# The last tile's output product with tokens on the partitions, in four banks, stored as rows of 1 KB

## What is computed

```python
X = np.fft.rfft(x, axis=1)
Yr = Xr @ w_r - Xi @ w_i + b_r
Yi = Xr @ w_i + Xi @ w_r + b_i
# each of both: sign(Y) * max(|Y| - 0.01, 0)
y = np.fft.irfft(Yr + 1j * Yi, n=3008, axis=1).reshape(12032, 256)
h = y @ w_in                                # 256 -> 2048
g = np.maximum(h, 0) + alpha * np.minimum(h, 0)
out = g @ w_out                             # 2048 -> 256
```

## Time and profile before

| | |
|---|---|
| median of 3 runs | 1376.64 us (1376.47 to 1377.29) |
| profiled execution, its own time | 1377.65 us |
| its span | 1375.8 us |
| TensorE busy | 1358.3 us, 99% of the span |
| VectorE, ScalarE, POOL busy | 1028.1, 765.3, 327.2 us |
| mean granted TensorE clock | 0.998 of full speed |

### The profile page before, as it was taken

How to read it: one execution, slowest core, us unless ns; L and a number is a source line. 1 busy time by engine, 2 the same in 40 slices (tenths; PEclk the granted TensorE clock), 3 DMA queues, 4 the chain that set the end, 5 groups by cost and what they waited for, 6 DMA issues and landing times.

```text
span 1375.8 us, 21743 instructions
## 1 busy us (share of the span) xinstructions
PE 1358.3 (99%) x6933; PEld 1157.8 (84%) x6933; DVE 1028.1 (75%) x1891; ACT 765.3 (56%) x1711; POOL 327.2 (24%) x370
## 2 busy tenths in 40 slices
PE   7999999999999999999999999999999999999997
PEld 5998888888888888888888888888888888888886
DVE  7877788898866768989866668888886666566654
ACT  4875566666544555655644546666564444444443
POOL 4534442232201422323300332233220000000000
PEclk9999999999999999999999999999999999999999
DMA  8754523231221541323302333223211021102101
GB/s 263 186 169 131 176 61 93 68 96 50 52 51 41 148 114 56 87 69 82 80 29 50 89 110 80 81 66 83 83 43 44 26 50 39 25 26 50 27 15 16
DMA packets 174892, 106.82 MB, mean 78 GB/s; under 512 B 112438, under 2 KB 150582, under 8 KB 174779
## 3 DMA queue, kind: packets, MB, share of 16 engines
q1 hardware_dynamic: 170340, 101.58, 27.6%
q10 hardware_dynamic: 3959, 3.70, 0.8%
q0 software_dynamic: 480, 0.16, 0.1%
HBM read 67.89 MB, written 37.49 MB: 77 GB/s over the span
## 4 chain that ended last, share of the span: by engine, by line
PE 96%; DVE 2%; DMA 1%; ACT 1%; issue 0%; POOL 0%; POOLq 0%; SPq 0%; DVEq 0%; ACTq 0%
PE out_ps L546 40%; PE h_ps L546 39%; PE work_ps L546 11%; PE work_ps L648 2%; PE work_ps L580 2%; PE work_ps L650 1%; PE work_ps L581 1%; DVE x_lo L1050 1%; DMA pair_raw<-fwd_scratch 1%; DVE x_hi L1058 0%; ACT above L881 0%; DMA x_raw<-in_x_dram 0%; DMA fwd_scratch<-g_raw 0%; DVE shrunk L1120 0%; ACT shr_hi L887 0%
## 5 line engine op out<-in xcount | busy, mean ns | idle before, releaser
L920 ACT ACTIVATE rows<-h_ps 128x502 f32<-128x502 f32 (+1 forms) x384 | 225.7, 588 | 509.8 <-PE h_ps L546 509.8
L1151 DVE SCALAR_TENSOR_TENSOR g_raw<-rows,keep,h_ps 128x502 f32<-128x502 f32 (+1 forms) x384 | 280.2, 732 | 264.3 <-ACT rows L920 260.4
L546 PE MATMUL out_ps<-g_hi,wout_hi 128*128 128x502 f32 (+1 forms) x768 | 305.0, 397 | 0.1
L546 PE MATMUL h_ps<-y_hi,win_hi 128*128 128x502 f32 (+1 forms) x768 | 300.4, 391 | 0.9 <-DVE y_lo L1050 0.9
L546 PE MATMUL h_ps<-y_lo,win_hi 128*128 128x502 f32 (+1 forms) x768 | 300.4, 391 | 0.0
L546 PE MATMUL out_ps<-g_hi,wout_lo 128*128 128x502 f32 (+1 forms) x768 | 299.8, 390 | 0.0
L546 PE MATMUL h_ps<-y_hi,win_lo 128*128 128x502 f32 (+1 forms) x768 | 299.5, 390 | 0.0
L546 PE MATMUL out_ps<-g_lo,wout_hi 128*128 128x502 f32 (+1 forms) x768 | 299.0, 389 | 0.0
L1050 DVE TENSOR_TENSOR g_lo<-g_raw,g_hi 128x502 fp32r<-128x502 f32 (+1 forms) x384 | 268.9, 700 | 1.8 <-ACT g_hi L929 1.4
L929 ACT ACTIVATE g_hi<-g_raw 128x502 fp32r<-128x502 f32 (+1 forms) x384 | 237.1, 617 | 6.6 <-DVE g_raw L1151 6.2
L546 PEld LDWEIGHTS h_ps<-y_hi,win_hi 128*128 128x128 f32 x768 | 145.4, 189 | 31.4 <-issue 1.0
(11 more groups left out here) (174 smaller groups left out, 2024.9 us busy)
## 6 DMA issues: line engine op xcount, KB each, us to landing
pair_raw<-fwd_scratch SPq DMA_DIRECT2D x96, 128.0 KB, 2.2
rows<-inv_scratch SPq DMA_DIRECT2D x61, 192.0 KB, 2.5
table<-in_twiddles_dram SPq DMA_DIRECT2D x28, 384.0 KB, 3.5
inv_scratch<-inv_sb SPq DMA_DIRECT2D x36, 256.0 KB, 2.2
x_raw<-in_x_dram SPq DMA_DIRECT2D x56, 160.0 KB
fwd_scratch<-staging SPq DMA_DIRECT2D x46, 192.0 KB, 2.1
inv_sb<-inv_scratch SPq DMA_DIRECT2D x122, 64.0 KB, 2.3
out_dram<-turned SPq DMA_DIRECT2D x124, 40.0 KB, 1.8
```

Source lines behind the costliest of these rows:

```text
L546: mm = pe.matmul(ps, lhs, rhs, start=(first and n == 0), stop=(last and n == len(terms) - 1), **kw)
L920: act.activation(negpart[:, q % 2, 0:size], h_ps[:, q % 2, 0:size], ACT.Relu, scale=-1.0).then_inc(negpart_done, 1)
L1151: dve.scalar_tensor_tensor(g_raw[:, q % 2, 0:size], negpart[:, q % 2, 0:size], keep[:, m:m + 1], h_ps[:, q % 2, 0:size], ALU.mult, ALU.add ...
```

## The change

Only the last tile's output product, its way out of the banks and its stores are changed. In `output_last` the weights of the array are blocks of g (124, 128, 128 and 120 tokens, by LAST_AT) and the moving operand is w_out, 256 features wide. So the tokens lie on the partitions and a token's 256 features in a row. Four banks collect the four blocks: the two of `out_ps` and the first two of `work_ps`. A step has twelve matmuls of 256 columns instead of six of 500. The wait for `g_lo` stands inside the first block, before its third matmul; the first two need `g_hi` alone. The waits for tile 22's transposes are at block 0 and block 1, and block 2 waits for the last reading of `work_ps` by the first layer.

Each block has its own signal in the last step. VectorE copies blocks 0 and 2, ScalarE blocks 1 and 3, into the place that `turned` has for this tile; there are no transposes for it. Eight transfers store whole rows of 1 KB, one transfer for each stretch of a block with one value of b: 30 and 94 rows (block 0, SP), 94 and 34 (block 1, POOL), 60 and 68 (block 2, SP), 26 and 94 (block 3, ScalarE).

```diff
+LAST_AT = (0, 124, 252, 380, 500)
+LAST_BLOCKS = len(LAST_AT) - 1
...
+def last_runs():
+    runs = []
+    for j in range(LAST_BLOCKS):
+        at = LAST_AT[j]
+        while at < LAST_AT[j + 1]:
+            b, a = divmod(TILE_AT[2][0] + at, NA)
+            count = min(NA - a, LAST_AT[j + 1] - at)
+            runs.append((j, at - LAST_AT[j], count, b, a))
+            at += count
+    return runs
...
+        out_rows_v = out.rearrange("(g a b) d -> g a b d", a=NA, b=NB)
...
+        def last_bank(j):
+            return out_ps[:, j, 0:DIM] if j < 2 else work_ps[:, j - 2, 0:DIM]
...
+        def store_last(eng, n, landed):
+            j, at, count, b, a = last_runs()[n]
+            eng.wait_ge((last_even, last_odd)[j % 2], j // 2 + 1)
+            eng.dma_start(out_rows_v[BATCH - 1, a:a + count, NB // 2 + b, :],
+                          last_place(j)[at:at + count, :]).then_inc(landed, 16)
...
-            for n in (0, 2, 4, 6):
-                store_out(sp, TILES - 1, n)
+            for n in (0, 1, 4, 5):
+                store_last(sp, n, last_stored)
...
-                sp.wait_ge(out_stored[k], 16 * (12 * TILES // 2 - 3 * k))
-            sp.wait_ge(out_handed, 16 * 3)
+                sp.wait_ge(out_stored[k], 16 * 12 * (TILES // 2 - k))
+            sp.wait_ge(last_stored, 16 * 6)
+            sp.wait_ge(out_handed, 16 * 2)
...
+            def output_last(m):
+                q = (TILES - 1) * STEPS + m
+                pe.wait_ge(g_hi_done, q + 1)
+                for j in range(LAST_BLOCKS):
+                    at = slice(LAST_AT[j], LAST_AT[j + 1])
+                    ps = last_bank(j)[0:LAST_AT[j + 1] - LAST_AT[j], :]
+                    gh, gl = g_hi[:, q % 3, at], g_lo[:, q % 3, at]
+                    hi, lo = wout_hi[:, m // 2, m % 2, :], wout_lo[:, m // 2, m % 2, :]
+                    if m == 0 and j < 2:
+                        pe.wait_ge(turned_done, 2 * (TILES - 1) - 1 + j)
+                    if m == 0 and j == 2:
+                        pe.wait_ge(biased_done, PAIRS * BATCH)
+                    product(ps, [(gh, hi), (gh, lo)], first=m == 0, last=False)
+                    if j == 0:
+                        pe.wait_ge(g_lo_done, q + 1)
+                    mm = product(ps, [(gl, hi)], first=False, last=m == STEPS - 1)
+                    if m == STEPS - 1:
+                        mm.then_inc(last_mm, 1)
+                if m < STEPS - 1:
+                    mm.then_inc(out_mm, 1)
...
-            for n in (1, 3, 5, 7, 8):
-                store_out(act, TILES - 1, n)
+            for j in range(1, LAST_BLOCKS, 2):
+                act.wait_ge(last_mm, j + 1)
+                act.wait_ge(out_stored[(TILES - 1) % 2], 16 * 12 * ((TILES - 1) // 2))
+                rows_of = slice(0, LAST_AT[j + 1] - LAST_AT[j])
+                act.activation(last_place(j)[rows_of, :], last_bank(j)[rows_of, :], ACT.Copy).then_inc(last_odd, 1)
+            for n in (6, 7):
+                store_last(act, n, last_stored)
...
-            turn(TILES - 1, 0)
-            turn(TILES - 1, 1)
+            for j in range(0, LAST_BLOCKS, 2):
+                dve.wait_ge(last_mm, j + 1)
+                dve.wait_ge(out_stored[(TILES - 1) % 2], 16 * 12 * ((TILES - 1) // 2))
+                rows_of = slice(0, LAST_AT[j + 1] - LAST_AT[j])
+                dve.tensor_copy(last_place(j)[rows_of, :], last_bank(j)[rows_of, :]).then_inc(last_even, 1)
...
-            for n in (9, 10, 11):
-                store_out(pool, TILES - 1, n, out_handed)
+            for n in (2, 3):
+                store_last(pool, n, out_handed)
```

More of the change, by code:

```diff
@@ L250, in mixer_kernel @@
         head_loaded, out_handed = sem("head_loaded"), sem("out_handed")
+        last_mm, last_even, last_odd, last_stored = (sem(n) for n in ("last_mm", "last_even", "last_odd", "last_stored"))
         ffw_loaded = [sem(f"ffw_loaded_{k}") for k in range(2)]
@@ L348, in mixer_kernel, with store_out @@
         wout_v = w_out.rearrange("(m p) e -> p m e", p=P)
+        out_rows_v = out.rearrange("(g a b) d -> g a b d", a=NA, b=NB)
         out_v = out.rearrange("(g a b) (h q e) -> g q a b h e", a=NA, b=NB, h=DH, q=4)
-        def store_out(eng, f, n, landed=None):
+        def store_out(eng, f, n):
             g, q, (k, b, count) = f // 6, n % 4, TILE_STORES[f % 3][n // 4]
@@ L357, in store_out, with last_place @@
                          turned[32 * q:32 * q + rows, f % 2, k, at:at + count, :, :].rearrange("p b h e -> p (b h) e")
-                         ).then_inc(landed or out_stored[f % 2], 16)
+                         ).then_inc(out_stored[f % 2], 16)
+        def last_bank(j):
+            return out_ps[:, j, 0:DIM] if j < 2 else work_ps[:, j - 2, 0:DIM]
+        def last_place(j):
+            return turned[:, (TILES - 1) % 2, :, :, :, :].rearrange("p k b h e -> p (k b h e)")[:, j * DIM:(j + 1) * DIM]
+        def store_last(eng, n, landed):
[3 more added lines that the diff above has]
+                          last_place(j)[at:at + count, :]).then_inc(landed, 16)
         def store_fwd(eng, s):
@@ L789, in _ @@
                     q = f * STEPS + m - LAG
-                    if q >= 0:
+                    if q >= (TILES - 1) * STEPS:
+                        output_last(q % STEPS)
+                    elif q >= 0:
                         output(*divmod(q, STEPS))
             for m in range(STEPS - LAG, STEPS):
-                output(TILES - 1, m)
+                output_last(m)
         @block.scalar
```

## The result

The changed kernel takes 1379.73 us (1378.97 to 1381.22, 14 runs), the kernel before 1377.47 us in the same jobs (1376.37 to 1378.41, 14 runs). The ratio is 1.0018, 95% interval 1.0011 to 1.0025: slower by 2.5 us (1.5 to 3.4). The forecast was +0.65 us, "no difference", and a time of 1377.3 in a range up to 1379.6.

A forecast was written before the change was run, and what follows sets the result against it. TensorE, busy 99%, bounds the kernel until the tail. The last data run starts 0.1 us sooner (+1.05 of longer steps paid back) and lasts +0.8: +0.65 after rounding on 1376.64 gives 1377.3 us, range 1374.3 to 1379.6.

The forecast's parts named there:

- The product: Last tile's output product: twelve 256-column matmuls take 1.43 us against 1.357, +0.075 a step, 13 steps +1.0 us, +0.05 at tile start.
- The handover to step 15: Before the last output product: the present 0.25 us wait for g_lo goes and nothing takes its place.
- Copies: Out of the banks: ScalarE 0.37 us and VectorE 0.42 us a copy; last block out 0.47 later, block 0 0.55 earlier.
- issues: Tail stores: an issue takes about 0.45 us on SP and ScalarE and 0.7 on POOL.
- The deal of the rows: Tail stores on SP and ScalarE: rows go to engines in equal shares, so 94 rows mean two engines with 47 each.
- the rival without it (1374.5): Tail stores: the 94-row stores are dealt over all 16 engines, 2.1 us sooner, 1374.5 us; chance 0.14.
- The price of a row: Tail data: 0.045 us a row, upper bound 0.055; 117 rows keep the first two engines busy 5.3 us, to 1375.2.
- POOL's rows: Tail stores: the main case (chance 0.58) counts only SP's and ScalarE's 119 rows on the first two engines, none of POOL's.
- the rival (+2.1): POOL's 94 rows fall on the same two engines, 47 more rows: +2.1 us, 1379.4, up to 1380.5; chance 0.22.
- The end: After the last data: landing comes 0.5 us behind and the span's end 0.75 later, as in the kernel before.
- the stretch at a low share: Sign in the tail: data moving at an eighth of 16 engines for some 4 us after 1371, where it was near nine.
- SP's last wait: Sign at the end: SP's wait for the last landing is around 5 us, against 4.0 in the kernel before.

The follow-up runs named there:

- The split version: The changed kernel with every 94-row store issued as 80 + 14 rows, eleven stores in place of eight: 1375.99 us, ratio to the kernel before 0.9988.

## Why the prediction was wrong

**The product: right, a little too dear.** Forecast 0.075 a step, measured 0.060, since twelve matmuls take 1.417 us and not 1.43. With the wait at block 1 (0.12 where I took 0.05) the output of step 13 starts 0.90 later, forecast 1.05. Weight loads of 124 and 120 columns cost nothing, as taken.

**The handover to step 15: right.** No wait for g_lo of any length; step 15 gains 0.15 on step 13's delay (0.90 to 0.75), where the forecast had 0.10 (1.05, less the 0.25 of wait, plus the 0.15 of the covering outputs).

**Copies: right; issues: shorter than taken.** VectorE's copy takes 0.42 as taken, ScalarE's 0.38 for 0.37. The last copy ends 0.31 later on the common scale (forecast 0.47). The first store is issued 0.71 earlier (forecast 0.55), and an issue takes SP 0.32 where I took 0.45. So the data begin 0.73 earlier, 0.18 more than forecast.

**The deal of the rows: right.** 94 rows are on two engines, 47 each; this was the step on which the forecast stood, and the rival without it (1374.5) is out. The split version, which has no such stores, comes to 0.9988 of the time before.

**The price of a row: the step that failed.** The prediction put "0.045 us a row", from a 256-row store over 16 engines, and 0.055 as upper bound. The runs with such a line of rows give 0.051 (one store alone), 0.055 (six stores in one queue) and 0.058 (the same six in two queues, as in the change). The forecast had 5.7 us from the first byte at 1369.5 to the last at 1375.2; the run without POOL's stores, which is the forecast's case, took 6.9: +1.2 us. The lone stores show why a mean is not enough: once it flows, a row takes 0.042 to 0.045, but for the first 1.3 us of the 94 rows the rate is about three quarters of that, and for the first 2.2 us of the 89 rows about three fifths. Why a packet takes longer then wasn't tried and stays open. My error was to take, between ends that differed by 1.2 us, the mean of a transfer in which each engine has 16 rows for one in which it has 117.

**POOL's rows: the second part of the error.** I left them out of the line of the first two engines in my own case and put 47 in the rival (+2.1). It is neither: about nine rows on each, and +0.6 measured. The rival's time, 1379.4, is near the measured 1379.73, but by another mechanism, so that is luck. Its upper end was also summed wrongly: 164 rows at 0.055 are 9.0 us, which gives 1381.1 and not 1380.5.

**The end: a third part.** From the data's end to the span's end are 1.5 us after and 1.25 before; 0.2 us.

Together 1.2 + 0.6 + 0.2, less the 0.18 of the earlier begin, are the 1.85 us by which +0.65 fell short of +2.5. Of the signs named, the stretch at a low share came, from 1372.5 on, against a share before of 0.73 to 0.89 and not throughout near nine; SP's last wait is 7.2 us, not around 5. The baseline in the new runs lay 0.8 higher as well (1377.47 for 1376.64), which moves the absolute time but not the ratio.

## What to carry to other kernels

What a transfer costs can hang on the divisors of its number of rows before it hangs on its bytes: on SP's and ScalarE's queues look for the largest number up to 16 that divides the slowest dimension, and split 94 into 80 + 14 rather than send it whole. The symptom in a profile is a tail at a busy share of one tenth and a steady low rate, and the number of packets under 512 B of a lone store on these two queues tells how many engines took part. A split has the price of an issue, here 0.3 to 0.4 us on its queue, so stop where the issues become the line.

## What the runs showed that I had not expected

That a lone store of 91 rows takes 0.6 us of data, one of 94 rows 2.4 and one of 89 rows 4.6 was expected from the deal once the change had been measured; the last two took longer than the 2.0 and the 3.8 to 4.5 expected. The same 94 rows from POOL take at most 0.6 us and land 2.1 us after the issue, since that queue deals them unequally over 16 engines. And an engine with a long line of rows runs its first 1.3 to 2.2 us below the rate that it reaches later: 17 to 18 GB/s with 47 rows, 10 to 18 with 89 (in half microseconds), against 24, though it counts as busy nearly all that time.
